# Chunked attention inside a two-layer MLP pass: four steps per group instead of three, and one instruction for the q and k blocks

## The reference

```python
scores = scale * np.matmul(q_c, k_c.transpose(0, 1, 2, 4, 3))   # q, k, v: (8, 8, 576, 64), chunks of 64
scores = scores - np.max(scores, axis=-1, keepdims=True)
attn = np.exp(scores)
attn = attn / (np.sum(attn, axis=-1, keepdims=True) + 1e-09)
out = np.matmul(attn, v_c)
...
x = np.ascontiguousarray(attn_out.transpose(0, 2, 1, 3)).reshape(B * S, H * D)
...
h = x @ w_in;  r = np.maximum(h, 0.0);  x = (r * r) @ w_out             # first MLP, 512 -> 2048 -> 512
...
h = x @ w_in;  g = np.where(h >= 1, h, np.where(h <= -1, 0, (h + 1) ** 2 / 4));  out = g @ w_out
```

## Time and profile before

| | us |
|---|---|
| median of 3 runs | 1710.74 |
| lowest and highest of the runs | 1708.66, 1711.58 |
| span of the profiled execution, first to last instruction | 1708.6 |
| PE busy | 1670.7 |
| DVE busy | 998.4 |
| ACT busy | 623.8 |

### The profile page before, as it was taken

One profiled execution on the slowest core, in us unless ns is written; L12 is line 12 of the kernel. 1 busy time (PEld: TensorE's weight loads), 2 busy tenths in 40 slices (PEclk: granted clock), 3 DMA queues, 4 the chain that ended last, 5 costly groups with the idle time before them and its releaser, 6 DMA issues.

```text
span 1708.6 us, 23067 instructions
## 1 busy us (share of the span) xinstructions
PE 1670.7 (98%) x8248; PEld 1370.4 (80%) x8248; DVE 998.4 (58%) x2223; ACT 623.8 (37%) x1476; POOL 42.9 (3%) x71
## 2 busy tenths in 40 slices
PE   6989999999999999999999999999999999999999
PEld 5768888888778878887888888888888888888887
DVE  5996958597695948869334444444443444343433
ACT  5554444444344434444454222222222222222222
POOL 1110000000000000000121000000000000000000
PEclk9999999999999999999999999999999999999999
DMA  7341111121111211111232010101010100001000
GB/s 155 111 112 44 38 50 42 33 56 38 46 38 55 45 27 56 38 44 28 96 99 99 1 50 1 50 1 49 0 49 0 38 12 24 25 17 33 5 21 25
DMA packets 126664, 74.76 MB, mean 44 GB/s; under 512 B 115552, under 2 KB 115552, under 8 KB 124256
## 3 DMA queue, kind: packets, MB, share of 16 engines
q1 hardware_dynamic: 121440, 56.64, 12.1%
q0 software_dynamic: 5120, 16.78, 3.2%
HBM read 54.53 MB, written 18.87 MB: 43 GB/s over the span
## 4 chain that ended last, share of the span: by engine, by line
PE 78%; DVE 18%; issue 2%; ACT 0%; DVEq 0%
PE h_ps L305 37%; PE acc L342 23%; PE acc L338 15%; DVE q_t L609 5%; DVE k_diag L609 5%; DVE v_and_probs_diag L652 3%; PE scores_ps L369 2%; DVE hidden_split L675 1%; PE heads_out_ps L400 1%; DVE score_max L628 1%; DVE x_t_split L590 1%; DVE probs L641 1%; DVE w_in_split L579 0%; DVE w_out_split L584 0%; PE h_ps L316 0%
## 5 line engine op out<-in xcount | busy, mean ns | idle before, releaser
L305 PE MATMUL h_ps<-x_t_split,w_in_split 128*128 128x512 f32 x3432 | 828.7, 390 | 6.8 <-issue 6.1
L305 PEld LDWEIGHTS h_ps<-x_t_split,w_in_split 128*128 128x128 f32 x3432 | 646.6, 188 | 142.6 <-issue 7.4
L338 PE MATMUL acc<-hidden_split,w_out_split 128*128 128x512 f32 x1728 | 421.8, 393 | 5.1 <-DVE hidden_split L675 5.1
L342 PE MATMUL acc<-w_out_split,hidden_split 128*128 128x512 f32 x1728 | 415.2, 389 | 0.9 <-DVE hidden_split L675 0.9
L338 PEld LDWEIGHTS acc<-hidden_split,w_out_split 128*128 128x128 f32 x1728 | 320.9, 188 | 79.8 <-issue 13.1
L342 PEld LDWEIGHTS acc<-w_out_split,hidden_split 128*128 128x128 f32 x1728 | 324.4, 188 | 68.5 <-ACT hidden_split L511 1.3
L675 DVE TENSOR_TENSOR hidden_split<-hidden_raw,hidden_split 128x512 fp32r<-128x512 f32 x288 | 199.4, 692 | 279.8 <-ACT hidden_split L511 277.7
L670 DVE SCALAR_TENSOR_TENSOR hidden_raw<-hidden_raw 128x512 f32<-128x512 f32 x144 | 99.6, 692 | 349.3 <-ACT hidden_raw L506 349.3
L511 ACT CAST hidden_split<-hidden_raw 128x512 fp32r<-128x512 f32 x288 | 178.7, 621 | 218.1 <-DVE hidden_raw L673 213.5
L501 ACT ACTIVATE hidden_raw<-h_ps 128x512 f32<-128x512 f32 x144 | 86.1, 598 | 441.2 <-PE h_ps L305 439.7
L506 ACT ACTIVATE hidden_raw<-h_ps 128x512 f32<-128x512 f32 x144 | 86.1, 598 | 367.6 <-PE h_ps L305 367.6
(11 more groups left out here) (57 smaller groups left out, 406.8 us busy)
## 6 DMA issues: line engine op xcount, KB each, us to landing
qk_in<-in_q_dram SPq DMA_DIRECT2D x72, 128.0 KB, 2.9
qk_in<-in_k_dram SPq DMA_DIRECT2D x72, 128.0 KB, 3.1
v_and_probs_diag<-in_v_dram SPq DMA_DIRECT2D x72, 128.0 KB, 2.9
mlp_out_t<-stage SPq DMA_DIRECT2D x9, 1024.0 KB, 3.9
v_and_probs_diag<-mlp_out_t SPq DMA_DIRECT2D x9, 1024.0 KB, 7.0
out_dram<-stage SPq DMA_DIRECT2D x8, 1024.0 KB, 5.0
stage<-in_moe_w_in_dram POOLq DMA_DIRECT2D x16, 256.0 KB, 4.1
stage<-in_moe_w_out_dram POOLq DMA_DIRECT2D x16, 256.0 KB, 4.1
```

The lines of the kernel that those rows point to most:

```text
L305: last = nc.tensor.matmul(h_ps[:, bank, :], w_in[:, kt, w, cols], x_t[:, par, x, kt, :], start=(kt == 0 and w == HI and x == HI), stop=(kt ...
L338: last = nc.tensor.matmul(acc[:, j, :], w_out[:, f, w, cols], hid[:, half, x, :], start=first, stop=end)
L342: last = nc.tensor.matmul(acc[:, j, :], hid[:, half, w, cols], w_out[:, f, x, :], start=first, stop=end)
```

## The change

- A group takes four steps (QUARTER = 4). PE visits attention at f = 3, 7, 11 and 15, each time with the head output of a group and then the score of the next one. The score at f = 15 belongs to the first group of the next tile, so the pipeline runs across the tile's edge. The first group of this pipeline (group 4) is scored at f = 0 of tile 0.
- `q_t` and `k_diag` become one buffer `qk_t` with three parts per pair of heads: q, k of the first head, k of the second (each padded with zeros in the other head's rows). One DVE instruction transposes a block of q and the same block of k: 16 instructions of 32x(4x2x32) for 32 of 32x(4x32). They are spread 3, 5, 4, 4 over four steps, those of the next group but one beginning in the step of the visit.
- `turn_probs` is split over two steps; the normalising moves to the step behind the visit.
- Group 4 is transposed by PE in the prologue, ahead of `up_half(1, 0)`, and copied by DVE ahead of the weights; the loads of its q and k move ahead of those of v for groups 2 and 3 on SP's queue.
- Tiles 6 and 7 are written out behind the loop, on PE, ACT and DVE, which now runs over tiles 2 to 5; the last group has no score behind it.

```diff
-AT_TURN, AT_SCORE, AT_PROBS, AT_PV = 0, 3, 4, 6
-CADENCE = 3
-TURN_SHARES = (10, 16, 32)
-
-
-def group_at(step, stage):
-
-    g, rest = divmod(step - stage, CADENCE)
-    return g if rest == 0 and 0 <= g < GROUPS else None
+QUARTER = 4
+EARLY = GROUPS + 1
+TURNS = (0, 3, 8, 12, 16)
...
-        q_t = sb("q_t", [P, HP, P])
-        k_diag = sb("k_diag", [P, HP, 2, 2, CHUNK])
+        qk_t = sb("q_t_and_k_t_by_head", [P, HP, 3, P])
...
+        def ends(t, g):
+
+            return isinstance(t, int) and GROUPS * (t + 1) + g >= NG
...
-                if not past(g, GROUPS + 2):
+                if not past(g, EARLY + 2):
                     if g >= 2:
                         sp.wait_ge(k_turned, g - 1)
                 else:
-                    sp.wait_ge(qk_turned, g - 1 - GROUPS)
+                    sp.wait_ge(qk_turned, g - 1 - EARLY)
...
             load_qk(3, 1)
+            load_qk(4, 0)
             load_v(2, 0)
             load_v(3, 1)
-            load_qk(4, 0)
...
-            pool.wait_ge(qk_turned, NG - GROUPS)
+            pool.wait_ge(qk_turned, NG - EARLY)
...
-                        last = nc.tensor.matmul(s_ps[rows, hp, :], q_t[:, hp, rows], k_diag[:, hp, c, :, :],
+                        last = nc.tensor.matmul(s_ps[rows, hp, :], qk_t[:, hp, 0, rows], qk_t[:, hp, 1:3, rows],
...
+                    if attends and not past(t, 1) and f == 0:
+                        score(GROUPS)
+                    if attends and f % QUARTER == QUARTER - 1:
+                        g = f // QUARTER
                         head_out(GROUPS * (t + 1) + g, g % 2)
-                    if attends and (g := group_at(f, AT_SCORE)) is not None:
-                        score(GROUPS * (t + 1) + g)
+                        if not ends(t, g + 1):
+                            score(GROUPS * (t + 1) + g + 1)
...
             turn_probs(GROUPS - 1)
+            turn(GROUPS)
             up_half(1, 0)
...
-            with pe.Fori(2, LAST_A, 2) as t:
+            with pe.Fori(2, LAST_A - 2, 2) as t:
                 tile(t, 0, 0, True)
                 tile(t + 1, 1, 0, True)
+            tile(LAST_A - 2, 0, 0, True)
+            tile(LAST_A - 1, 1, 0, True)
             tile(LAST_A, 0, 0, False)
...
-                blocks = [(which, tok, wid) for which in range(2) for tok in range(4) for wid in range(4)]
-                for which, tok, wid in blocks[begin:end]:
-                    src = qk_in[tok * BLK:(tok + 1) * BLK, par, which, :].rearrange(
-                        "t (hp wid e) -> t hp wid e", hp=HP, e=BLK)[:, :, wid, :]
-                    rows = slice(wid * BLK, (wid + 1) * BLK)
-                    if which == 0:
-                        dst = q_t[rows, :, tok * BLK:(tok + 1) * BLK]
-                    else:
-                        c, at = tok // 2, tok % 2 * BLK
-                        dst = k_diag[rows, :, c, wid // 2, at:at + BLK]
+                blocks = [(tok, wid) for tok in range(4) for wid in range(4)]
+                for tok, wid in blocks[begin:end]:
+                    src = qk_in[tok * BLK:(tok + 1) * BLK, par, :, :].rearrange(
+                        "t a (hp wid e) -> t hp a wid e", hp=HP, e=BLK)[:, :, :, wid, :]
+                    head = wid // 2
+                    dst = qk_t[wid * BLK:(wid + 1) * BLK, :, 0:head + 2:head + 1, tok * BLK:(tok + 1) * BLK]
                     last = nc.vector.transpose(dst, src)
...
-            def turn_probs(n):
-
-                dve.wait_ge(normed, n + 1)
-                dve.wait_ge(headed, n)
+            def turn_probs(n, part):
+
+                if part == 0:
+                    dve.wait_ge(normed, n + 1)
+                    dve.wait_ge(headed, n)
                 heads = probs[:].rearrange(by_head, n=CHUNK)
-                for tok in range(4):
+                for tok in (2 * part, 2 * part + 1):
                     for wid in range(2):
-                        at = tok // 2 * CHUNK + wid * BLK
+                        at = part * CHUNK + wid * BLK
                         last = nc.vector.transpose(probs_diag[at:at + BLK, :, tok * BLK:(tok + 1) * BLK],
                                                    heads[tok * BLK:(tok + 1) * BLK, :, wid * BLK:(wid + 1) * BLK])
-                last.then_inc(probs_turned, 1)
+                if part == 1:
+                    last.then_inc(probs_turned, 1)
...
-                    if attends and (g := group_at(f, AT_TURN + CADENCE - 1)) is not None:
-                        turn(GROUPS * (t + 1) + g, g % 2, TURN_SHARES[-2], TURN_SHARES[-1])
-                    if attends and (g := group_at(f, AT_PROBS)) is not None:
-                        turn_probs(GROUPS * (t + 1) + g)
-                    if attends and (g := group_at(f, AT_SCORE)) is not None:
-                        find_max(GROUPS * (t + 1) + g)
+                    g, r = divmod(f, QUARTER)
+                    n = GROUPS * (t + 1) + g
+                    begins = not past(t, 1) and f == 0
+                    if attends and (r == 0 and not begins or not past(t, 1) and f == 1):
+                        normalise(n)
+                    if attends and r in (1, 2):
+                        turn_probs(n, r - 1)
+                    if attends and r == 3 and not ends(t, g + 1):
+                        find_max(n + 1)
...
+                    if attends and begins:
+                        find_max(n)
...
-                    if attends and (g := group_at(f, AT_PV)) is not None:
-                        x_in_lo(GROUPS * (t + 1) + g, 1 - par, g)
-                    for part in range(CADENCE - 1):
-                        if attends and (g := group_at(f, AT_TURN + part)) is not None:
-                            turn(GROUPS * (t + 1) + g, g % 2, (0, *TURN_SHARES)[part], TURN_SHARES[part])
-                    if attends and (g := group_at(f, AT_SCORE)) is not None:
-                        normalise(GROUPS * (t + 1) + g)
+                    if attends and r == 3:
+                        x_in_lo(n, 1 - par, g)
+                        if not ends(t, g + 2):
+                            turn(n + 2, g % 2, TURNS[0], TURNS[1])
+                    if attends and r < 3 and not ends(t, g + 1):
+                        turn(n + 1, (g + 1) % 2, 0 if begins else TURNS[r + 1], TURNS[r + 2])
...
+            copy_qk(GROUPS)
```

More of the change, by code:

```diff
@@ L119, in build_program @@
         out_ps = ps("heads_out_ps", [P, HP, P])
-        ident_zero, ident_ready, k_diag_zero, probs_diag_zero, spare_zero = map(
-            sem, ("ident_zero", "ident_ready", "k_diag_zero", "probs_diag_zero", "spare_zero"))
+        ident_zero, ident_ready, k_zero, probs_diag_zero, spare_zero = map(
+            sem, ("ident_zero", "ident_ready", "k_zero", "probs_diag_zero", "spare_zero"))
         w_in_loaded = [sem(f"w_in_loaded{i}") for i in range(2)]
@@ L359, in score @@
             def score(n):
-                if past(n, GROUPS):
-                    pe.wait_ge(qk_turned, n + 1 - GROUPS)
+                if past(n, EARLY):
+                    pe.wait_ge(qk_turned, n + 1 - EARLY)
                 else:
@@ L511, in tile @@
                     nc.scalar.copy(hid[:, half, HI, :], raw[:, half, :]).then_inc(hid_hi, 1)
-                    if attends and (g := group_at(f, AT_PV)) is not None:
+                    if attends and not past(t, 1) and f == 0:
+                        exponentials(GROUPS)
+                    if attends and f % QUARTER == QUARTER - 1:
+                        g = f // QUARTER
                         x_in_hi(GROUPS * (t + 1) + g, 1 - par, g)
-                    if attends and (g := group_at(f, AT_SCORE)) is not None:
-                        exponentials(GROUPS * (t + 1) + g)
+                        if not ends(t, g + 1):
+                            exponentials(GROUPS * (t + 1) + g + 1)
                     if f == 0 and past(t, 1):
@@ L556, in _ @@
             tile(1, 1, 0, True)
-            with act.Fori(2, LAST_A, 2) as t:
+            with act.Fori(2, LAST_A - 2, 2) as t:
                 tile(t, 0, 0, True)
                 tile(t + 1, 1, 0, True)
+            tile(LAST_A - 2, 0, 0, True)
+            tile(LAST_A - 1, 1, 0, True)
             tile(LAST_A, 0, 0, False)
@@ L617, in copy_qk @@
                     dve.wait_ge(scored, g)
-                nc.vector.tensor_copy(q_t[:].rearrange("p hp n -> p (hp n)"), acc[:, 0, :])
+                nc.vector.tensor_copy(qk_t[:, :, 0, :], acc[:, 0, :].rearrange("p (hp n) -> p hp n", hp=HP))
                 dve.wait_ge(k_turned, g + 1)
@@ L621, in copy_qk @@
                     rows = slice(head * D, (head + 1) * D)
-                    last = nc.vector.tensor_copy(k_diag[rows, :, :, head, :], acc[rows, 1, :].rearrange(
-                        "p (hp c n) -> p hp c n", hp=HP, c=2))
+                    last = nc.vector.tensor_copy(qk_t[rows, :, 1 + head, :], acc[rows, 1, :].rearrange(
+                        "p (hp n) -> p hp n", hp=HP))
                 last.then_inc(qk_copied, 1)
@@ L708, in split_x @@
```

(8 more changed lines are left out.)

## The result

| | before | changed |
|---|---|---|
| median, us | 1710.31 (4 runs) | 1685.13 (4 runs) |
| lowest and highest | 1708.66, 1711.58 | 1684.29, 1686.10 |
| ratio | | 0.9854, 95% interval 0.9840 to 0.9868 |
| span of the profiled execution | 1708.6 | 1684.3 |

Faster by 25.2 us. The profiled execution of the changed kernel took 1686.1 us, 1.8 more than its span, and every execution on record here is 1.7 to 2.4 us longer than its span. So it was chance that the span of before, 1708.6, agreed with the lowest of its runs, and that span doesn't say that its execution was 2.1 us faster than the median. The forecast took a difference of spans, which this leaves as it is.

A forecast was written before the change was run, and what follows sets the result against it. PE, busy 98% of the span, bounds the kernel, with DVE full during attention. Savings of 6.6 us (prologue, tile 0) and 14.0 (5.7 jump, 8.3 visits and late scores) give 1710.7 - 20.6 = 1690.1 us, range 1685 to 1698.

The forecast's parts named there:

- The joint transpose at 436 ns: DVE's 16 transposes of 256 elements take 436 ns each, replacing 32 of 303 ns; DVE saves 2.7 us a group.
- Case B: Rival: transposes cost 0.54 to 0.62 us, steady tiles stay free, tile 0 runs late; 1692.5 to 1698 us, chance 0.12.
- Four steps, no late scores in tiles 1 to 7: Steady tiles: slack 1.9 us at the score, a tile 95.64 us, 8.3 us saved from visits and late scores.
- C: Rival at tile edges: the added score's maximum delays the next tile's first "up"; 1692.5 to 1694 us, chance 0.09.
- E: Rival: the order leaves the late scores, 0.45 us each for 31 scores, 14 us; 1704 us, chance 0.04.
- D: Rival: written-out tiles need fetching too, so the saved jump comes back, plus 5.7 us; 1696 us, chance 0.07.
- What matters is the order inside: DVE's order within a group's four steps: at most 4.75 of 5.44 us between low halves, never late, slack 1.9 us.
- Prologue and tile 0: Start to head output at f = 15 of tile 0: 131.2 us against 137.78, 6.6 saved; first head output near 58.5.
- v isn't held up: SP's queue: moving group 4's q and k loads ahead of v loads for groups 2 and 3 costs nothing.
- I price it 5.7, between 5.1 and 6.2, since its body holds as many PE instructions as before.: The one jump back left in the loop over tiles costs 5.7 us; dropping the other saves 5.7.
- Behind the last head output: After tile 7's last head output nothing changes, 0 us.

The follow-up runs named there:

- a_split: Changed kernel with q and k blocks transposed by an instruction each (32 of 128 elements) in its four steps; 1692.48 us, 7.4 above the changed kernel.
- b_unroll: Kernel before with only tiles 6 and 7 written out behind the loop on PE, ACT and DVE; 1702.88 us against 1706.99, ratio 0.9973.
- b_joint: Kernel before in its own three steps a group, with only the joint transposes of q and k added; 1691.40 us, ratio 0.9904.
- after_again: The changed kernel unaltered, run and profiled again later on another experiment's chip; 1684.95 us (1684.52 to 1685.18, 4 runs).
- b_pad64: Kernel before with 16 small products (64 more PE instructions) ahead of the first transpose, shifting the loop; 1700.46 us, ratio 0.9956.
- a_pad208: Changed kernel with 52 small products on PE in the prologue, shifting the loop; 1688.85 us (2 runs), 3.7 above the changed kernel.
- a_pad192: Changed kernel with 48 small products on PE in the prologue, 32 ahead of the first transpose and 16 ahead of the first score; 1685.90 us.

## Why the prediction was right, and where it was not

*The joint transpose at 436 ns.* Right to the digit. The 0.54 us by the fixed part of 58 cycles in the table of the Trainium skill, page "VectorE: DVE Perf Modes", section on the TRN2 errata, did not come; the measurement decides for the trace's larger fixed part of 0.17 us. The same section says below its table that the fixed part as measured is about 150 cycles, an estimate of 0.16 us at 0.96 GHz, and with that the trace agrees; I had taken only the table. Case B is left as an experiment: a_split cost 7.4 where I had expected 6 to 9 for it, though not all of it where I had it.

*Four steps, no late scores in tiles 1 to 7.* Right: DVE 15.60 us a group where I had 15.6, tiles of 95.52 us where I had 95.64 (a visit with both is 2.12, not 2.15). Cases C and E did not happen, nor did D: there is no issue wait in tiles 6 and 7, here or in b_unroll. But the step "What matters is the order inside" gave the credit to four steps together with the joint transposes; b_joint shows that the joint ones alone do it. I had not worked out three steps with the smaller work: 17.63 - 2.7 = 14.9 us in 18.4, which is what b_joint measures.

*Prologue and tile 0.* 5.4 saved for 6.6. The first head output came at 59.89 for my 58.5, and all of that is there at the first "down" already, 44.87 for 43.5. PE had waited 1.54 us for the load for group 3, which I had costed at nothing ("v isn't held up" was so, k was). That load isn't all of it either: after_again waits 1.43 for it and still has its first head output at 58.59, since its rows ahead of the wait come 1.1 earlier. From the first "down" on the working was right: the third "up" 5.08 behind it for my 5.1, held by DVE's eight transposes as I had it, the first score 0.59 late instead of 1.0, then none.

*The step that failed: "I price it 5.7, between 5.1 and 6.2, since its body holds as many PE instructions as before."* It measured 0.83. Here the number of instructions in the loop is not what counts, its place is. I took two prices of one program for a property of the jump. b_pad64 and a_pad208 show it from both sides: 0.95 and 0.6 in the kernel before, 5.2 in the changed one. Of the term's 4.9 us error, some 2 to 3 belong to the clock, which had fallen at both jumps of the execution that I read; in b_unroll and b_joint it fell at one jump of three.

*Behind the last head output* I had nothing and it is 0.9 longer: at the two jumps back of phase B's loop (near 1154 and 1328 us) PE's products come 0.35 and 0.52 late where in before they come on time. This too goes with the place of the loop: a_pad192 and a_pad208, the same kernel behind more filler, are back at 881.6. Between 1160 and 1530 us the large instruction queue has 17 DMAs in the changed kernel, and one each in before and in a_pad192.

*The range* held by 0.1 us, and that was luck: the runs of the changed kernel lie on both sides of 1685, and their later median, 1684.95, is below it. The range did not have in it that a jump could be nearly free; with 1 us as the lowest price of the one that is left it would have reached some 4 us lower.

## What to carry to other kernels

- When an engine that trails the bound one is full, compute its work per step after each part of a change by itself. Here merging two small instructions into one of twice the size was enough, and stretching the schedule as well bought the steady tiles nothing but paired visits (2.6 us), while the start as rebuilt for it cost 5.1 us.
- "Issue" in a list of waits isn't always a wait for instructions. Before you price it, see what the other engines finish just before it ends: the 2.12 us at the third "up" ended 0.1 behind a write of DVE.
- A stall at a loop's jump back can be one of placement. A few instructions of filler, hidden in a wait that is there anyway, move it; look at whether the wait stands before or a few instructions behind the loop's first instruction. Any edit ahead of a loop can give or take those microseconds, and a comparison of two kernels should subtract them.

## What the runs showed of the hardware that was not expected

- PE's wait at a jump back depends on where the loop starts: 2.2 to 2.8 us behind one product, 0.34 behind nine, none further on, beside 0.3 to 1.0 ahead of the first. The same program moved by 64 instructions went from 11.4 us for two jumps to 1.5 in the two profiled executions, and by 6.5 us in the median of its runs.
- After PE had stood idle for 2.1 to 2.9 us the granted clock sometimes fell to the lower level of 1.2 GHz and sometimes not: 11 products behind the jump took 4.19 us in before and 2.68 in b_unroll, which is the same program up to there, and the third "up" of the changed kernel was slow in one execution and not in the other. What decides it stays open. In the changed kernel the window below shows it at the start of tile 0; the "up" took 4.57 us, but the "down" behind it had to wait for DVE in any case (4.41 us from one to the next, 4.21 in the execution where the clock stayed), so the fall cost 0.2 us.

```profile
50.00:53.40 3.40, 3.40 (x8) 2.72 (x9) 3.24 (x9) 2.00 (x4) 1.28 (x2) 0.51 0.44 147
```
